# Chunk-selected attention and a gated MLP: a written order for every engine, and chunk bounds of four heads on eight 64x32 tiles

## The reference, cut to what matters

```python
# q, k, v: (4, 8, 768, 64); 24 chunks of 32 keys
ub = sum_d max(q * k_min[chunk], q * k_max[chunk])      # bound per query and chunk
ub = where(causal, ub, -1e9); top = argsort(ub)[..., -6:]
scores = where(chunk selected and causal, q @ k.T / 8, -1e9)
attn = softmax(scores) @ v
x = attn as (4, 768, 512)                               # 4 batches, 8 heads of 64
h = gelu_tanh(x @ w_in); u, g = halves of h             # w_in: 512 x 1024
g = layernorm(g) * g_ln
g = w_sg @ g + b_sg                                     # w_sg: 768 x 768, over positions
out = x + (u * g) @ w_out                               # w_out: 512 x 512
```

## Time and profile before

| | |
|---|---|
| runs | 267.54, 264.81, 267.44 us; median 267.44 |
| profiled execution, first to last instruction | 262.9 us; 4.5 us under the median of the runs |
| PE busy | 225.0 us, 86% |
| DVE busy | 197.7 us, 75% |
| ACT busy | 153.4 us, 58% |
| POOL busy | 76.9 us, 29% |
| chain that ended last | PE 50%, DVE 32%, ACT 9% |

### The profile page before, as it was taken

The page is one execution under the profiler, slowest core; times in us unless marked ns, Lnnn a source line. Parts: engine busy times, 40 slices in busy tenths (PEclk is TensorE's granted clock), DMA queues, the critical chain, the costliest instruction groups (busy, mean ns, idle before and its releaser), DMA issues.

```text
span 262.9 us, 5801 instructions
## 1 busy us (share of the span) xinstructions
PE 225.0 (86%) x2242; PEld 140.2 (53%) x2258; DVE 197.7 (75%) x561; ACT 153.4 (58%) x232; POOL 76.9 (29%) x99
## 2 busy tenths in 40 slices
PE   8886488987996599998899899997998998689874
PEld 3444256665743378655555577566445765434431
DVE  6949579787558668989677988886588876467883
ACT  1444848977649545655784974658757645846000
POOL 3353728653201424222212433134210211202000
PEclk9999689999999569999999999999999999999999
DMA  7999999998999904856751443122101031100033
GB/s 167 201 225 202 205 221 197 235 227 175 199 209 160 212 19 109 228 132 182 163 122 43 100 100 135 51 95 55 38 6 24 2 122 58 64 0 0 0 123 120
DMA packets 84652, 32.39 MB, mean 123 GB/s; under 512 B 77232, under 2 KB 80912, under 8 KB 84624
## 3 DMA queue, kind: packets, MB, share of 16 engines
q1 hardware_dynamic: 82608, 29.26, 48.1%
q0 software_dynamic: 2016, 2.75, 6.4%
HBM read 24.77 MB, written 6.29 MB: 118 GB/s over the span
## 4 chain that ended last, share of the span: by engine, by line
PE 50%; DVE 32%; ACT 9%; issue 6%; POOL 1%; POOLq 1%
PE PSG L794 9%; PE PSG L814 8%; PE PSC L677 8%; PE PSG L613 7%; DVE W L546 5%; ACT E L682 5%; DVE vhat L767 5%; PE PSG L751 4%; PE PSG L696 4%; DVE vsT L801 3%; PE PSG L777 3%; DVE uT L805 3%; DVE m_1 L629 2%; DVE XS L713 2%; PE PSC L463 2%
## 5 line engine op out<-in xcount | busy, mean ns | idle before, releaser
L682 ACT ACTIVATE E<-PSC 128x1024 bf16<-128x1024 f32 (+1 forms) x96 | 84.5, 920 | 44.7 <-PE PSC L677 44.1
L686 POOL TENSOR_SCALAR_AFFINE_SELECT E<-E 128x768 bf16<-128x768 bf16 x32 | 28.5, 892 | 59.9 <-ACT E L682 59.6
L794 PE MATMUL PSG<-wsgT,vhat 128*128 128x384 bf16 x192 | 36.6, 335 | 4.9 <-DVE vhat L767 3.0
L546 DVE TENSOR_REDUCE W<-PSG 128x12 f32<-128x384 f32 x64 | 33.1, 543 | 7.5 <-PE PSG L540 7.3
L677 PE MATMUL PSC<-QB,KB 128*128 128x128 bf16 (+1 forms) x224 | 26.0, 253 | 2.7 <-ACT E L682 2.7
L677 PE MATMUL PSC<-QA,KA 88*128 88x128 bf16 (+1 forms) x224 | 24.8, 249 | 3.4 <-ACT E L682 2.6
L794 PEld LDWEIGHTS PSG<-wsgT,vhat 128*128 128x128 bf16 x192 | 18.3, 100 | 17.6 <-DVE vhat L767 3.0
L801 DVE SCALAR_TENSOR_TENSOR vsT<-PSG,glnT,bsgbc 128x384 f32<-128x384 f32 x32 | 19.7, 614 | 7.6 <-PE PSG L794 7.5
L814 PE MATMUL PSG<-woutb,uT 128*128 128x512 bf16 x88 | 21.8, 380 | 3.9 <-DVE uT L805 3.3
L777 PE MATMUL PSG<-xT,winb 128*128 128x384 bf16 x128 | 23.8, 327 | 0.4 <-DVE xT L727 0.3
L696 PE MATMUL PSG<-vx,E 128*128 128x65 bf16 x480 | 20.4, 195 | 4.1 <-ACT E L682 2.7
(11 more groups left out here) (69 smaller groups left out, 343.7 us busy)
## 6 DMA issues: line engine op xcount, KB each, us to landing
kn<-in_k_dram SPq DMA_DIRECT2D x32, 192.0 KB, 3.6
qn<-in_q_dram SPq DMA_DIRECT2D x32, 192.0 KB, 3.6
vn<-in_v_dram SPq DMA_DIRECT2D x32, 192.0 KB, 3.5
out_dram<-osb SPq DMA_DIRECT2D x24, 256.0 KB, 2.0
vgb<-in_moe_w_sg_dram POOLq DMA_DIRECT2D x6, 192.0 KB, 5.9
QB<-QA SPq DMA_DIRECT2D x12, 96.0 KB, 2.2
KB<-KA SPq DMA_DIRECT2D x12, 96.0 KB, 3.0
winb<-in_moe_w_in_dram POOLq DMA_DIRECT2D x4, 256.0 KB, 5.9
```

The costliest lines, as they stand in the source:

```text
L546: P.op("dve", lambda d, t=t, m=m, op=op, hf=hf: d.tensor_reduce(W[w][:, m, 12 * hf:12 * hf + 12], t.ap()[:, 0:TG].rearrange("p (c x) -> p ...
L682: P.op("act", lambda e, t=t, c0=c0, c1=c1: e.activation(E[es][:, c0:c1], t.ap()[:, 0:c1 - c0], ACTF.Exp, scale=SCALE), act(c1 - c0), reads ...
L686: P.op("pool", lambda g: g.affine_select(ev, ev, pattern=[[0, NT], [1, 128]], compare_op=ALU.is_ge, fill=0.0, base=0, channel_multiplier=- ...
L794: r = e.matmul(t.ap()[:, 0:TG], vhat[s][:, sb, 128 * fb:128 * fb + 128], wsgT[:, sb, TG * tg:TG * tg + TG], start=(sb == 0), stop=(sb == N ...
```

## The change

The work on paper stays the same; nearly every function is touched. The planner, its costs and its priorities are gone. A table names every operation of every engine (`sc.1.0@0` is the first score piece of head 1 in PSUM bank 0), gives the order, the PSUM bank and the number of filler matmuls (`+6`). PSUM is one tensor of eight banks: scores in banks 0 and 2 (two banks each), all else in banks 4 to 7 without further restriction.

- k and q of a pair are transposed into two banks at once; each is then read out by one instruction over both (two reductions for k instead of four, one copy for q instead of two). ACT writes `KA` and `KB` directly for all pairs, and POOL casts q twice per pair; the 36 DMAs of lines 563, 565 and 594 are gone.
- Groups for the selection are pair 0, pair 1, and then seven groups of two pairs. The bound matmuls of a group of two pairs write both halves of the queries, one to a bank, the second half with the column groups swapped (`j ^ 2`), so that all eight matmuls of a step lie on different 64x32 parts of the array. A single pair does the same with its two heads on four parts. One DVE transposition takes both banks.
- Selected rows go on by eight DMAs of 24x288 instead of four of 24x768; in the two single groups by four DVE transpositions.
- `XS` has another layout, and for batches 1 to 3 `xT` comes from a transposing DMA on SP instead of six PE matmuls and a DVE copy.
- The loads of `b_sg` and `g_ln` move from the fifth and sixth DMA of SP to head 4. The negative number in the indicator is larger.

```diff
-    def schedule(self):
...
-    def fill(self, until, fn):
...
+GROUPS = [[0], [1]] + [[i, i + 1] for i in range(2, 16, 2)]
+DIRECT = ()
+XDMA = (1, 2, 3)
+SWAP = 1
+
+TABLE = {
+    "pe": """
+    c.idle kt.0@4+6 qt.0@6+2 kt.1@6+2 ub1.0@4+1 qt.1@4+1 kt.3@6 qt.2@4 qt.3@4+2 sc.1.0@0 sc.1.2@2 kt.2@6 ub1.1@4
...
+            t = P.tile(2, ANY2)
+
+            def ub(e):
+                for m in range(2):
+                    for hf in range(2):
+                        for j, (w, i) in enumerate(heads):
+                            lo, c = 64 * i, 32 * (j ^ (2 * hf * SWAP))
+                            rhs = qT[w][lo:lo + 64, LO + HSEL * hf:LO + HSEL * (hf + 1)] if m == 0 else \
+                                rT[w][lo:lo + 64, HSEL * hf:HSEL * (hf + 1)]
+                            r = e.matmul(t.ap()[c:c + 32, 512 * hf:512 * hf + HSEL], W[w][lo:lo + 64, m, :], rhs,
+                                         start=(m == 0), stop=(m == 1), tile_position=(lo, c))
+                return r
+            P.op(f"ub2.{g}", "pe", ub, reads=rd, alloc=t)
+            P.op(f"u2.{g}", "dve", lambda d: d.transpose(
+                Uf.rearrange("p (h x) -> p h x", h=2),
+                t.ap().rearrange("p (h x) -> p h x", x=512)[:, :, 0:HSEL]), writes=[("U", u)], ps=[t])
...
         def xtrans(b, dk):
-            t = ps_g.tile((0, 1, 2) if b == 0 else (0, 1))
+            rd = [("XS", b % 2, dk, 0), ("XS", b % 2, dk, 1)]
+            if b in XDMA:
+                P.op(f"xd.{b}.{dk}", "sp", lambda e: e.dma_start_transpose(
+                    xT[b % 2][:, dk, :].rearrange("p (j x) -> p j x", x=128),
+                    XS[:, b % 2, dk].rearrange("p j x -> p (j x)")),
+                    reads=rd, writes=[("xT", b % 2, dk)], dma=f"x{b % 2}_{dk}")
+                return
+            t = P.tile(1, ANY)
...
-        P.schedule()
-        P.fill(min(o.start for o in P.ops if o.ps and o.ps[0].slot == 1 and o.ps[0].cls is ps_score) - 1.0, idle)
+        order, banks, fill = unpack(TABLE, P)
+        P.place(order, banks, fill)
         P.link()
-        P.emit(nc, ctx)
+        P.emit(nc, ctx, idle)
```

More of the change, by code:

```diff
@@ new lines, in unpack, with __init__ @@
+def unpack(table, P):
+    at = {o.name: o.idx for o in P.ops}
+    order, bank, fill = {}, {}, {}
+    for e in ENGINES:
+        order[e] = []
+        for w in table[e].split():
+            w, _, n = w.partition("+")
+            w, _, b = w.partition("@")
+            i = at[w]
+            order[e].append(i)
+            if b:
+                bank[P.ops[i].alloc.idx] = int(b)
+            if n:
+                fill[i] = int(n)
+    return order, [bank[t.idx] for t in P.tiles], fill
+class Tile:
+    def __init__(self, psum, idx, banks, where):
+        self.psum, self.idx, self.banks, self.where = psum, idx, banks, where
+        self.bank = None
+        self.ops, self.runs = [], []
@@ L49, with tile @@
 class Program:
     def __init__(self):
[L55 to L58, removed]
+        self.ops, self.tiles = [], []
+        self.writer, self.readers, self.dma_sems = {}, {}, {}
+        self.psum = None
         self.base = 0.0
[L61 to L78 removed]
+    def tile(self, banks, where):
+        t = Tile(self.psum, len(self.tiles), banks, where)
+        self.tiles.append(t)
+        return t
@@ new lines, in place @@
+    def place(self, order, banks, fill):
+        self.order, self.filler = order, fill
+        for t, b in zip(self.tiles, banks):
+            t.bank = b
+        owner = {}
+        for i in order["pe"]:
+            t = self.ops[i].alloc
+            if t is None:
+                continue
+            for b in range(t.bank, t.bank + t.banks):
+                if b in owner:
+                    for x in owner[b].ops:
+                        self.ops[i].deps[x.idx] = True
+                owner[b] = t
+        flight = []
+        for i in order["sp"]:
+            if self.ops[i].bulk:
@@ L235, in schedule @@
-        self.busy = {e: sum(ops[i].cost for i in order[e]) for e in ENGINES}
-        self.seq = sorted(range(len(ops)), key=lambda i: (ops[i].start, ops[i].pos))
-    def fill(self, until, fn):
-        self.filler = {}
-        end = 1.5
-        for i in self.order["pe"]:
-            o = self.ops[i]
-            if o.start > until:
-                break
-            n = int((o.start - end - 0.25) / 0.23)
-            if n > 0:
-                self.filler[i] = n
-            end = max(end, o.end)
-        self.filler_fn = fn
+        last = None
@@ L252, in link @@
+        for i in order["pool"]:
+            if self.ops[i].dma is not None:
+                continue
+            if last is not None and (last.lane or self.ops[i].lane):
+                self.ops[i].deps[last.idx] = True
+            last = self.ops[i]
+        for e in ENGINES:
+            for n, i in enumerate(order[e]):
+                self.ops[i].pos = n
     def link(self):
```

842 lines of the change are left out of this document (396 added, 446 removed).

## The result

The changed kernel takes 234.4 us (median of 4 runs, 232.4 to 236.4) against 267.4 before: ratio 0.877, 95% interval 0.871 to 0.883. The forecast was 239.0, the range 226 to 258. The profiled execution spans 232.5 us, 2.4 us under the forecast span of 234.9. The forecast added 4.5 us to its span for what lies around it. On record a run of 234.27 us has a span of 232.5, and a run of the kernel before with the same span of 262.9 us takes 264.58: what lies around it is 1.7 to 1.8 us, and the other 2.7 us of the 4.5 are a difference between runs. About half of the 4.6 us by which the forecast is too high is that.

The account below looks back on a forecast made before the run. No engine was full throughout; PE (50% of the chain of waits) and DVE (32%) set the end. Span 262.9 - 11 - 9 - 5 - 6 + 3 = 234.9 us, with 4.5 to the median 239 us; range 226 to 258.

Parts of the forecast that it names:

- The start, -11: Up to the twelfth exponential: first exponential at about 18 us, four heads end at about 35; -11 us, bounds -6 and -17.
- The middle and the hole: 46 to 229 us: -9 us, from 12.6 us of PE work leaving; hole at 73 to 100 us: -5 us.
- Bound matmuls, -6.6 of PE: Selection's bound groups: eight matmuls go at once, so a double group takes 1.10 us; 6.6 us saved after the start.
- rival 2: Bound matmuls: the second half goes after the first; 6 us more, 245; chance 0.12.
- Transposing DMAs, 6.0 us of PE and 6.6 of DVE off, +3 for waits: Batches 1 to 3: 72 of 96 transposing matmuls and 12 of 16 copies go; 4 us per DMA, waits +3 us.
- Reductions, -3 us of DVE: DVE: 64 reductions at 543 ns become 32 at 988; 34.8 us become 31.6, bounds 0 and -17.
- The hole at 73 to 100 us, -5: 73 to 100 us: PE need not idle for `vhat`, other heads' work standing in between; -5 us, bounds 0 and -8.
- The tail, 37 us instead of 34: After the last head: batch 2's mixing and output matmuls move there; 37 us, stretch before 9 shorter, together -6 us.
- (1): DVE becomes the bound: busy 75% of the time as now, span 249, time 254; chance 0.17.
- (3): Transposing DMAs hold the SP queue and the MLP waits; at 20 us each, 281 us; chance 0.10.
- (4): The written order does not fit the real durations; the start alone is won, 261 us; chance 0.08.
- the signs named: Exponentials near 18 and 35 us; double group 1.1; transposing DMAs 3 to 5; clock near 1 from 60; tail 37.

Follow-up runs that it names:

- experiment 4: Changed kernel with batches 1 to 3 transposed on PE again, with DVE copies and no transposing DMA, all else in the same order: 245.9 us.
- experiment 2: Changed kernel with each two-bank reduction of k split into two of 384 columns, under the same order: 234.4 us.
- Experiment 8: Changed kernel with v of pairs 3 to 15 not loaded (26 of 96 loads leave the SP queue): 230.5 us.
- experiments 7 and 10: Changed kernel with SP-queue loads moved ahead of the selection's DMAs: in 7 as early as buffers are free, 238.8 us; in 10 only five loads, 237.8 us.
- experiment 3: Changed kernel's operations ordered by a list planner with estimated costs instead of the table: 277.2 us, ratio to the kernel before 1.044.
- experiment 1: Changed kernel with the second query half of the bound matmuls back in the same column groups as the first: 235.4 us.

## Why the prediction was right, and which steps were not

*The start, -11*: the first exponential was put at 18 us and the twelfth at 35; they came at 18.27 and 34.95 against 46.05, -11.1. Right at that place, but not all of the lead lasted: at the 24th exponential 4.8 us of it are left, some 7 with the work done ahead. The sum carried all 11 through to the end.

*The middle and the hole.* From the twelfth exponential to the last product with v the prediction took off 9 + 5 and 9 more that move to the tail, and added 3: 20 us. The stretch went from 229.43 - 46.05 = 183.4 us to 194.70 - 34.95 = 159.8, 23.6 less, although the next 12 exponentials took 6.3 us longer than before, some 2 of them for work done ahead. The sum held, but its terms did not, so that it came so near is in part luck:

- *Bound matmuls, -6.6 of PE.* The price was right: eight go at once, 1.14 us for a double group. The Trainium skill ("TensorEngine Tiling (Array Packing)", Gotcha 1: PSUM Pressure), by which row tiles do not write one bank at once, is not borne out by these fp32 matmuls. Of the -9 for 12.6 us of PE, some 4.7 are theirs; rival 2 put 6 on them, more than the sum holds. Undone they cost about 1 us, since four of seven groups stand where PE is not the limit. The step that failed is the one that spread PE's share evenly over the time from 46 to 229 us.
- *Transposing DMAs, 6.0 us of PE and 6.6 of DVE off, +3 for waits.* Undone they cost 11.5 us. The 4 us assumed for one were 2.8, and the wait charged at 1 us a batch was 0.2 us once. PE's part counts in full late, and with it go the waits between PE and DVE (6.4 and 6.8 us in experiment 4), which the prediction put at nothing. This is the term that was mis-sized most: 6.0 of the 12.6 us that made the -9, some -4, plus the 3 charged, about -1 in all, against -11.5. The estimate worked out from the 1309 ns that the Trainium skill gives for 128x128 ("VectorE: DVE Perf Modes", The three transpose paths), 7.9 us, is nearly three times what landed.
- *Reductions, -3 us of DVE*: 948 ns against 988 worked out; worth nothing that experiment 2 can tell from zero.
- *The hole at 73 to 100 us, -5.* This step failed. PE no longer waits for `vhat`, but between 35 and 85 us it idles 7.0 us of 50 (sums of the table) where it idled 7.8 from 46 to 100 us before, and the clock dips twice. What idle time went, went later: 5.3 us from 85 to 196 us, 10.1 from 100 to 229 before. The DMA share of 1.00 and 1.07 up to 73 us stood in the last columns of the earlier trace rows, and I did not read it: that stretch waits in part for loads. Experiment 8 shows it for some 3 to 4 us; experiments 7 and 10 show that two other orders of the queue don't help. The rest of that idle time is not traced to a cause.

What is left of the gain, 19.5 us with the three operations undone, is in part the start: there the twelfth exponential ends at 35.8, 10 us earlier than before, and the 24th at 54.8, 6.7 earlier.

```profile
51.53 3.25 ACT L670 ACTIVATE E<-PS 128x1024 bf16<-128x1024 f32 x4
```

So some 7 to 10 us are the start's. The other 10 to 13 come behind it, from the written order and the smaller parts (groups for the selection, two banks at a time, ACT's direct writes, 36 DMAs fewer). Which of these, no run here parts; experiment 3 shows only that the operations without a fitting order lose.

*The tail, 37 us instead of 34*: 37.8 instead of 33.5, with PE busy for 31.14 us of the last 37 instead of 25.41 of the last 34. Right.

*Rivals.* DVE did not stay at 75% but is busy for 82% of the span, and more work for it cost nothing measurable in experiment 2 (1). The second half does not go after the first (2). The transposing DMAs made PE wait for 0.2 us in all (3). The written order fits (4). Of the signs named, the start, the double group and the tail came as said; one did not come: the granted clock is not near 1 from 60 us on, but 0.93 from 60 to 85 us.

## What to carry to other kernels

Read the busy share of PE, DVE and DMA for every stretch before crediting removed work: in experiment 1 a microsecond of PE's work was worth a microsecond where PE was 95% busy and nothing measurable where it idled between waits. A lead won at the start has to be followed further: here a good part of it was gone twelve exponentials later. Work that passes to and fro between two strictly ordered queues can cost its own time on the busier one and the waits as well, so moving it to a third (here a transposing DMA) can win both. A dip of the clock and a load that comes last show where a wait is, not what would remove it; try both before building on them.

## What the runs showed of the hardware

A transposing DMA of 128x768 bf16 within SBUF lands in 2.8 us and holds its issuing queue for 1.28 us. Eight fp32 matmuls of 288 columns (shown as sixteen) on eight different 64x32 parts take 0.51 us until the next kind starts (59.93 to 60.44); on four parts, two on each, 0.99 us (59.51 to 60.50). Filling PE's gaps kept the granted clock up (0.99 instead of 0.96 and 0.97); the 24th exponential came 1 to 3 us earlier, and the time did not change by more than the runs can tell.
